# Attention, mixture of experts and Fourier mixing on one core: bounds read on one partition, the first group loaded in parts, tile 1 split earlier

## The reference

```python
# 1. attention, 8 heads of 64; a key is kept if it is one of the first n_global,
#    or lies up to n_local - 1 positions behind the query
keep = (pos < n_global) | ((rel >= 0) & (rel < n_local))
scores = where(keep, q @ k.T / 8 - slope[h] * dist, -1e9)
x = softmax(scores) @ v
# 2. one expert of 8 per token; a token may take over its predecessor's expert
e = argmax(x @ w_gate) if s == 0 or sigmoid(x @ w_local) < 0.5 else e_of_the_token_before
x = softmax(x @ w_gate)[e] * (relu(x @ w1[e]) @ w2[e])       # 512 -> 1024 -> 512
# 3. real part of a 2-d Fourier transform, normalisation, a 512 -> 2048 -> 512 block
u = x + real(fft(fft(x, axis=1), axis=2))
out = u + relu(norm(u) @ w_ch1) @ w_ch2
```

## Time and profile before

| | us |
|---|---|
| median of 3 runs | 669.6 (668.3 to 672.01) |
| the profiled execution's own time | 670.89 |
| its span, first to last instruction | 669.0 |
| PE busy | 645.6 |
| DVE busy | 315.9 |
| POOL busy | 213.9 |
| ACT busy | 210.0 |
| mean granted clock of PE | 0.992 of full speed |

### The profile page before, as it was taken

The page is one execution under the profiler, slowest core; times in us unless marked ns, Lnnn a source line. Parts: engine busy times, 40 slices in busy tenths (PEclk is TensorE's granted clock), DMA queues, the critical chain, the costliest instruction groups (busy, mean ns, idle before and its releaser), DMA issues. The chain is left out here.

```text
span 669.0 us, 10426 instructions
## 1 busy us (share of the span) xinstructions
PE 645.6 (96%) x3354; PEld 526.9 (79%) x3355; DVE 315.9 (47%) x829; ACT 210.0 (31%) x414; POOL 213.9 (32%) x120
## 2 busy tenths in 40 slices
PE   8999999888999999999998999999999999999997
PEld 6777887666888888887876778888888888888886
DVE  4999888576563453553547764541121112211112
ACT  3566454222333333333205453232111122111110
POOL 0000000334897967997535466260000000000000
PEclk9999999999999999999999699999999999999999
DMA  8797543324676765876344034100010000100001
GB/s 299 272 330 271 199 147 133 112 81 150 212 253 204 244 211 172 275 247 206 132 141 138 1 131 152 64 31 1 1 63 1 0 1 1 63 1 0 1 1 63
DMA packets 35906, 83.72 MB, mean 125 GB/s; under 512 B 3474, under 2 KB 7826, under 8 KB 35860
## 3 DMA queue, kind: packets, MB, share of 16 engines
q1 hardware_dynamic: 19024, 43.34, 18.4%
q10 hardware_dynamic: 14916, 33.47, 14.9%
q0 software_dynamic: 1920, 6.29, 3.0%
HBM read 67.36 MB, written 15.73 MB: 124 GB/s over the span
## 5 line engine op out<-in xcount | busy, mean ns | idle before, releaser
L752 POOL TENSOR_TENSOR w<-raw,w 128x1024 fp32r<-128x1024 f32 x56 | 132.5, 2401 | 30.2 <-ACT w L851 30.2
L1849 DVE SCALAR_TENSOR_TENSOR act_t<-psum,act_t 128x512 fp32r<-128x512 f32 x48 | 33.2, 691 | 190.1 <-ACT act_t L1150 190.1
L851 ACT ACTIVATE w<-raw 128x1024 fp32r<-128x1024 f32 x64 | 67.4, 1058 | 101.9 <-PE psum L613 40.3
L1150 ACT ACTIVATE act_t<-psum 128x512 fp32r<-128x512 f32 x48 | 28.7, 598 | 216.3 <-PE psum L613 216.3
L611 PE MATMUL psum<-un_t,wc 128*128 128x512 f32 x192 | 74.8, 390 | 1.4 <-DVE un_t L1776 1.4
L611 PE MATMUL psum<-wc,act_t 128*128 128x512 f32 x192 | 75.6, 394 | 0.0
L613 PE MATMUL psum<-wc,act_t 128*128 128x512 f32 x192 | 74.8, 390 | 0.0
L612 PE MATMUL psum<-wc,act_t 128*128 128x512 f32 x192 | 74.8, 389 | 0.0
L612 PE MATMUL psum<-un_t,wc 128*128 128x512 f32 x192 | 74.7, 389 | 0.0
L613 PE MATMUL psum<-un_t,wc 128*128 128x512 f32 x192 | 74.7, 389 | 0.0
L924 ACT ACTIVATE prob<-prob,top 128x256 f32<-128x256 f32 (+1 forms) x96 | 46.2, 482 | 49.7 <-DVE top L1488 49.3
(11 more groups left out here) (286 smaller groups left out, 1109.6 us busy)
## 6 DMA issues: line engine op xcount, KB each, us to landing
raw<-in_moe_w ACTq DMA_DIRECT2D x56, 512.0 KB, 4.2
k_win<-in_k SPq DMA_DIRECT2D x8, 768.0 KB, 7.3
raw<-in_moe_w_ch SPq DMA_DIRECT2D x12, 512.0 KB, 3.3
v_win<-in_v SPq DMA_DIRECT2D x8, 704.0 KB, 5.6
xs<-x_sorted SPq DMA_DIRECT2D x17, 256.0 KB, 4.1
raw<-in_moe_w SPq DMA_DIRECT2D x8, 512.0 KB, 8.4
y_sorted<-ys SPq DMA_DIRECT2D x16, 256.0 KB, 3.3
q_t<-in_q SPq DMA_DIRECT2D x8, 384.0 KB, 5.7
```

The lines of the kernel that those rows point to most:

```text
L752: nc.gpsimd.tensor_tensor(w[:, slot, 1, m, at_:at_ + PIECE], raw[:, n % RING, :], w[:, slot, 0, m, at_:at_ + PIECE].bitcast(f32), ALU.subt ...
L851: nc.scalar.activation(w[:, slot, 0, m, at_:at_ + PIECE], raw[:, n % RING, :], ACT.Copy).then_inc(high_done, 1)
L1150: nc.scalar.activation(act_t[n % 2][:, 0, :], bank(act_bank(n)), ACT.Relu).then_inc(act_high, 1)
L1849: nc.vector.scalar_tensor_tensor(act_t[n % 2][:, 1, :], bank(act_bank(n)), 0.0, act_t[n % 2][:, 0, :].bitcast(f32), ALU.max, ALU.subtract) ...
```

## The change

- **Bounds.** Each is loaded into one partition only. DVE makes `choice` there. PE, after 8 warm-up products instead of 24, multiplies a row of ones with the two numbers, which spreads them over the 128 partitions in PSUM; DVE copies them from there. 12 more warm-up products follow on PE.
- **Group 0.** Queries, keys and values come in three parts of two tiles each, nine loads for three, and PE's waits name the part. The host lays the values out so that a part is one stretch (tile `i` at `2 i`, its window at `2 i - 1`).
- **Weight pieces.** Piece 0 of expert 0 stays where it was; piece 1 is issued behind group 1's keys, pieces 2 and 3 behind its values.
- **Clears.** One semaphore counts all nine.
- **Tile 1.** On DVE, `x_tile(1, 1)` comes right behind `control`; placing, shares and first results follow it, and the two register loads come after tile 0's result. On PE, 9 fillers stand ahead of tile 1's turning, and the wait on the control numbers with one filler stands behind tile 0's last products.

```diff
@@ laid_out
-    v_win[:, :, 0:ST] = v_tiles
+    v_win[:, :, 0::2] = v_tiles
...
-            v_win[:, 0:GLB, ST + i - 1] = v_tiles[:, 0:GLB, 0]
-            v_win[:, GLB:P, ST + i - 1] = v_tiles[:, GLB:P, i - 1]
+            v_win[:, 0:GLB, 2 * i - 1] = v_tiles[:, 0:GLB, 0]
+            v_win[:, GLB:P, 2 * i - 1] = v_tiles[:, GLB:P, i - 1]
@@ sync
-            load_keys(0, q_loaded[0], k_loaded[0])
+            def first_group_keys(p):
+                sp.dma_start(q_t[0][:, 2 * p * P:(2 * p + 2) * P], ...
+                             ).then_inc(first_keys[p], 16)
+                sp.dma_start(k_win[0][:, 2 * p:2 * p + 2, :]...
+                             ).then_inc(first_keys[p], 16)
+            def first_group_values(p):
+                i0, i1 = max(4 * p - 1, 0), 4 * p + 3
+                sp.dma_start(v_win[0][:, i0:i1, :]...).then_inc(first_values[p], 16)
+            first_group_keys(0)
             sp.dma_start(square[:, :], a["c_square"]).then_inc(square_loaded, 16)
-            load_values(0, v_loaded[0])
+            first_group_values(0)
+            for p in range(1, ST // 2):
+                first_group_keys(p)
+                first_group_values(p)
             sp.dma_start(gate_w[:, :, :], a["gate"]).then_inc(gate_loaded, 16)
-            for n in range(RING):
+            def first_piece(n):
                 sp.dma_start(raw[:, n, :], ...).then_inc(raw_loaded[n], 16)
+            first_piece(0)
...
                 load_keys(1, q_loaded[1], k_loaded[1])
+                first_piece(1)
                 load_values(1, v_loaded[1])
+                for n in range(2, RING):
+                    first_piece(n)
...
-            sp.wait_ge(heads_cleared, 16 * CLEAR_STEPS)
-            sp.wait_ge(results_cleared, 16 * CLEAR_STEPS)
+            sp.wait_ge(cleared, 16 * (2 * CLEAR_STEPS + 1))
@@ gpsimd
-            pool.wait_ge(first_tile_cleared, 16)
+            pool.wait_ge(cleared, 16 * (2 * CLEAR_STEPS + 1))
@@ scalar
-                act.dma_start(bounds_i[:, 2 * n:2 * n + 2], a[name].bitcast(i32).unsqueeze(0).broadcast_to([P, 2])
+                act.dma_start(bounds_i[:, 2 * n:2 * n + 2], a[name].bitcast(i32).unsqueeze(0)
                               ).then_inc(bounds_loaded, 16)
@@ vector
-            link(nc.vector.tensor_copy(bounds[:, :], bounds_i[:, 0:4:2]))
+            nc.vector.tensor_copy(bounds_row[:, :], bounds_i[:, 0:4:2]).then_inc(bounds_ready, 1)
+            dve.wait_ge(bounds_ready, 1)
...
+            dve.wait_ge(bounds_spread, 1)
+            link(nc.vector.tensor_copy(bounds[:, :], bank(6)[:, 0:2]))
...
             control()
-            place_results()
-            share(1)
-            first_results()
-            half = HALVES_LEAST + nc.vector.value_load(ctl[0:1, CTL_MORE], ...)
-            odd = nc.vector.value_load(ctl[0:1, CTL_ODD], ...)
...
             x_tile(1, 1)
+            place_results()
+            share(1)
+            first_results()
             first_tile_result()
+            half = HALVES_LEAST + nc.vector.value_load(ctl[0:1, CTL_MORE], ...)
+            odd = nc.vector.value_load(ctl[0:1, CTL_ODD], ...)
             x_tile(2, 0)
@@ tensor
-            warm_up(24)
+            warm_up(8)
+            pe.wait_ge(bounds_ready, 1)
+            nc.tensor.matmul(bank(6)[:, 0:2], ones[0:1, :], bounds_row[:, :], start=True, stop=True
+                             ).then_inc(bounds_spread, 1)
+            warm_up(12)
...
-            keep_busy(6)
-            pe.wait_ge(ctl_ready, 1)
-            keep_busy(5)
+            keep_busy(9)
...
             turn_tile(1, 1, 16)
             for c in range(NF - 2, NF):
                 second_product(0, 0, c)
+            pe.wait_ge(ctl_ready, 1)
+            keep_busy(1)
             first_up(1, 1)
```

More of the change, by code:

```diff
@@ L171, in build @@
     gate_w = keep("gate_w", [P, NC, E + 1])
-    bounds_i = keep("bounds_i", [P, 4], i32)
+    bounds_i = keep("bounds_i", [1, 4], i32)
+    bounds_row = keep("bounds_row", [1, 2])
+    choose = keep("choose", [1, 3])
     bounds = keep("bounds", [P, 2])
@@ L381, in build @@
         choice_ready = sem("choice_ready")
+        bounds_ready = sem("bounds_ready")
+        bounds_spread = sem("bounds_spread")
         dve_chain = sem("dve_chain")
@@ L667, in _ @@
             with nc.sync.Else():
+                for n in range(1, RING):
+                    first_piece(n)
                 sp.dma_start(cdense[:, :, :].rearrange("p a n -> p (a n)"), a["c_dense"]).then_inc(g_dist, 16)
-                sp.wait_ge(q_loaded[0], 16)
-                sp.wait_ge(k_loaded[0], 16)
-                sp.wait_ge(v_loaded[0], 16)
+                for p in range(ST // 2):
+                    sp.wait_ge(first_keys[p], KEYS_FIRST)
+                    sp.wait_ge(first_values[p], VALUES_FIRST)
                 with sp.Fori(0, B * HP) as group:
@@ L1679, in _ @@
             x_tile(1, 1)
+            place_results()
+            share(1)
+            first_results()
             first_tile_result()
+            half = HALVES_LEAST + nc.vector.value_load(ctl[0:1, CTL_MORE], min_val=0, max_val=SLOTS // 2 - HALVES_LEAST)
+            odd = nc.vector.value_load(ctl[0:1, CTL_ODD], min_val=0, max_val=1)
             x_tile(2, 0)
@@ L2033, in scores @@
                     c0 = P if i == 0 else 0
-                    if i == 0:
-                        pe.wait_ge(q_loaded[r], 16 * (g // 2 + 1))
-                        pe.wait_ge(k_loaded[r], 16 * (g // 2 + 1))
+                    if g == 0 and i % 2 == 0:
+                        pe.wait_ge(first_keys[i // 2], KEYS_FIRST)
+                    if g > 0 and i == 0:
+                        pe.wait_ge(q_loaded[r], (KEYS_FIRST if r == 0 else 16) + 16 * (g // 2))
+                        pe.wait_ge(k_loaded[r], (VALUES_FIRST if r == 0 else 16) + 16 * (g // 2))
                     if n >= 2:
@@ L2059, in values @@
                     pe.wait_ge(prob_t_ready, n + 1)
-                    if i == 0:
-                        pe.wait_ge(v_loaded[r], 16 * (g // 2 + 1))
+                    if g == 0 and i == 0:
+                        pe.wait_ge(first_values[0], VALUES_FIRST)
+                    if g == 0 and i % 2 == 1 and i < ST - 1:
+                        pe.wait_ge(first_values[i // 2 + 1], VALUES_FIRST)
+                    if g > 0 and i == 0:
+                        pe.wait_ge(v_loaded[r], (VALUES_FIRST if r == 0 else 16) + 16 * (g // 2))
                     if n > 0:
@@ L2112, in _ @@
                     for n in range(3):
-                        pe.wait_ge(g_loaded[n], 16 * group + 16)
+                        pe.wait_ge(g_loaded[n], 16 * group + G_FIRST[n] + 16)
                     for i in range(ST):
```

38 lines of the change are left out of this document (22 added, 16 removed).

## The result

| | before | after |
|---|---|---|
| median us of 4 runs | 670.53 (668.3 to 672.01) | 663.55 (662.16 to 664.4) |
| ratio after to before, 95% | | 0.9898 (0.987 to 0.9926) |
| the profiled execution's own time | 670.89 | 663.25 |
| its span | 669.0 | 661.4 |
| mean granted clock of PE in it | 0.992 | 0.997 |

The changed kernel is faster by 7.0 us in the medians and by 7.6 in the two profiled executions; 664.0, and 6.1 less, had been predicted. Lines of the changed kernel are some 30 to 40 higher than before: L1211 the cast of the bounds, L1221 their copy out of PSUM, L1512 the bias, L1521 the score reduction, L1906 warm-up, L1911 the bounds product, L2079 scores, L1985 fillers, L1992 the turning of tiles, L618 to L620 the products in three passes, L1662 and L1664 the split of a tile, L881 ACT's weights, L782 POOL's.

The account below looks back on a forecast made before the run. PE, busy 96% of the span, was taken as the bound, leaving only its pauses and filler to win. Start -3.1 and tile 1 -3.0 made -6.1: 664.8 on the profiled basis, 663.5 on the median's; 664.0 named, range 661 to 668.3.

Parts of the forecast that it names:

- The sum: Whole kernel: start -3.1 and tile 1 -3.0 both reach the end, -6.1 us together.
- Part 1: Start: bounds on one partition land at 3.9, so the window distances start at 5.4 for 8.49, -3.1 us.
- PE's scores started at 9.72 and waited, so PE is not what is late: Start: the claim, from the old profile, that DVE's chain decides there, with the first score reduction at 12.44.
- The product is hidden by the choice chain: Start: PE's product spreading the bounds costs nothing, as 8 warm-ups end at 4.4 and the choice stands at 5.1.
- Late constants: Rival at the start: slopes stay late or bounds land well above 3.9; gain 0.8 to 2, about 666.5; chance 0.15.
- the large end: Start: upper end of the bounds gain, -3.9, if window constants also land up to 0.8 us earlier.
- Parts 2 and 3: Start: group 0 two tiles at a time, and three weight pieces behind group 1; each at no cost.
- Part 4: Tile 1 split right behind the control numbers: its first product at 157.4 for 160.50, rounded to -3.0 us.
- that rival: Tile 1: PE's two register loads in front of the first product cost in the open, gain 1.8, 665.2; chance 0.12.
- Part 5: Behind tile 1: placing, shares and first results end 2.2 us later, ACT starts at 160.4; covered, no cost.
- its rival: Expert weights: an unbroken chain from expert 1 to PE's late wait would absorb 5.2 us, giving 669; chance 0.07.
- A low clock into attention: Rival at the start: a warm-up break delays the clock's rise, about 1.5 us per unit, 676 with 8; chance 0.05.

Follow-up runs that it names:

- start_alone: The changed kernel with the tile 1 part undone; median 667.41 us against 669.88 before, -1.7 ±0.7 at equal clock.
- split_behind: The changed kernel with DVE's order at tile 1 undone, PE's kept; median 665.71 us against 665.65 before, -2.3 ±0.7 at equal clock.
- short_again: The changed kernel with 5 warm-up products for 12 behind the bounds product, run on the third chip; median 659.06 us against 665.65 before.
- bounds_alone: The kernel before with only the bounds on one partition and the clears on one semaphore; median 671.35 us against 669.88, +0.2 ±0.7 at equal clock.
- fewer_fillers: The changed kernel with 4 fillers for 9 in front of tile 1's turning; median 660.01 us against 665.65 before, -5.2 ±0.8 at equal clock.
- short_gap_filled: The changed kernel with 5 warm-up products for 12 and fillers in PE's pauses ahead of the mixing; median 658.31 us against 665.65 before.
- short_warm_up: The changed kernel with 5 warm-up products for 12 behind the bounds product, on the second chip; median 661.52 us against 669.78 before.
- tile1_alone: The kernel before with the tile 1 part of the change alone; median 666.12 us against 669.88, -3.6 ±0.6 at equal clock.
- after_again: The changed kernel itself in more executions, on the second chip; median 663.6 us against 669.78 before, -5.8 ±0.6 at equal clock.
- no_fill_behind: The changed kernel without the four fillers behind scores 1; median 665.5 us against 669.78 before, -5.0 ±0.6 at equal clock.

## Why the prediction was right, and where it was not

- **The sum**, -6.1 on the profiled execution: at equal clock -5.8 ±0.6, in the medians -7.0 in the first runs and -6.2 in the second. That the sum fits is in part luck, as two misses cancel: the start gave less than its 3.1, tile 1 more than its 3.0. That the time fits, 664.0 for 663.55, is luck as well. Before's median, 669.6 when the forecast was made, had become 670.53 with one more run, and the four executions of the changed kernel had a mean clock of 0.996, where the next six had 0.9943: by the slope 0.7 us.
- **Part 1, bounds, -3.1: the term that was too large.** On DVE it came as said: the landing at 3.9 at 4.02, the distances at 5.4 at 5.51, the first reduction near 9.3 at 9.49 and 9.25. In the times the whole start gave 1.7 ±0.7 (start_alone) and 2.3 ±0.7 (split_behind, whose tile 1 gains nothing); at unit 20 it was 2.2 to 3.1 in five profiles. Three of the five have 2.9 or more there, near the forecast; why the times show less than these marks is open. The step that failed is "PE's scores started at 9.72 and waited, so PE is not what is late". That held for the old order. The prediction took DVE's chain for all of the start and costed the warm-up only as cover, "done at 4.4" (it ended at 4.8), without asking when the 24 passes behind the bounds product end. With a late rise of the clock they end at 8.9, and scores 2 behind them are late by 0.6. "The product is hidden by the choice chain" failed too, by less: DVE's copy waited 0.18 us for it in the first profile and 0.66 in short_again. Of the start 0.27 more is lost between units 2 and 3 in each kernel with the new bounds (bounds_alone -0.02, then +0.25); why is open.
- **Late constants.** The 0.8 of early window constants at the large end was not won: cwin took 3.2 for 4.6, and nothing waited for it. Crow landed at 6.7 in the first profile, not late. In others it landed as late as 7.9, and the first reduction then came at 9.78 (fewer_fillers) and 9.91 (short_gap_filled). So late constants cost 0.3 to 0.4 us in those two, where the rival took 1.1 to 2.3 off part 1.
- **Parts 2 and 3, at zero.** Right that the start would run into group 1's keys without part 3, and that with it they don't delay it (16.3 against 17.9). The runs show what the prediction left unsaid: the start's gain belongs to the three together. Bounds alone give +0.2 ±0.7; without part 3, 2.6 are lost, without part 2, 1.3. Parts 2 and 3 by themselves were not run. PE waited for keys 0 in two of the profiles with part 2, 0.20 and 0.74 us; what that cost is not told apart. The Trainium skill's figure for the transfer that keeps the DMAs full (DMA: Bandwidth & Descriptors, "Why a DMA increments its semaphore by 16 and not by 1"), by which q's pieces would have taken 0.6 longer by the prediction's estimate, is neither borne out nor refuted: in short_warm_up PE began scores 0 at 7.13 without a wait, in short_again at 7.60 and in short_gap_filled at 8.09 with one.
- **Part 4, -3.0.** 3.35 in the first trace, 3.25 in tile1_alone's, 3.6 ±0.6 in its times, 3.5 ±0.9 by split_behind. Turn to product took 2.31 us for 2.5, so the register loads were hidden, and that rival fell. PE's reordering alone gives nothing (split_behind); DVE's alone was not run. Behind tile 1 the shift grew from 5.4 to 6.1 us, which the prediction did not name (a turning of hidden rows at 195.51 came at 189.40), and was back at 5.4 by the one at 306.73 (301.35).
- **Part 5, moved behind.** ACT started at 158.29, where 160.4 less the start was said. "At 199.43 ACT waits for PE again" was right in kind: it does at 207.44 and 232.03, and PE paid 0.3 late in the mixture (1.0 for 0.7), 0.6 in after_again (1.3). So the chain of weights absorbed a little, of the 5.2 that its rival named.
- **A low clock into attention.** It did not come in the changed kernel's profiles, but others have it: no_fill_behind, bounds_alone, and tile1_alone, which had before's start. The prediction priced it per unit, 1.5 us; in no_fill_behind 3.4 us at half clock (from its two stretches) cost 1.3 at unit 20 against after_again.
- **Not foreseen at all**: that single executions differ by 0.44 us for each 0.001 of mean clock. The profiled pair alone would have given the change 7.6 us, nearly 2 more than it is worth at equal clock.

## What to carry to other kernels

An early chain gives only what the next late one lets through: list for each start-up consumer when its data, its bias and its own engine are ready, and move them together: the bounds alone were worth nothing here (+0.2 ±0.7), and taking out either companion lost 1.3 or 2.6 us. List the engine that was waiting before too: it can be the late one once the chain ahead of it is short. Put the operation that another engine waits for directly behind what it needs, and bookkeeping behind it. Where the clock varies between executions, set times against the granted clock before reading a difference of less than one per cent.

## What the runs showed of the hardware

- PE's granted clock fell from 1.00 to 0.50 (2.4 to 1.2 GHz) behind three-us stretches with 1.69, 1.75 and 1.96 us of work and single pauses of 0.5 to 1.3 us, and stayed there for 3.4 to 10.2 us. Other profiles had such pauses, and a clock of 1.00 behind them. Longer pauses don't settle it either: in front of the gate's products near 123 us PE idled 2.18 us in before's profile and 2.14 in short_warm_up's without a fall, and 2.30 and 2.62 in start_alone and after_again with one. The Trainium skill (TensorE: Matmul & The Clock Gate, "What's actually happening") lets activity lift the clock and idling lower it; the direction agrees with the rows.
- The first rise comes at a different moment each time: 24 warm-up passes took 2.94 or 3.70 us in two executions of the same kernel.
- A load of eight bytes into one partition was there 2.7 us after its issue (1.3 to 4.02) where the same spread over 128 partitions took 6.2, and the loads beside it came sooner too: crow 5.1 for 8.1 (3.8 to 6.3 over all profiles with the new bounds), cwin 3.2 for 4.6.
